# Windowed attention and a gated product on one core: the fifth pass of the first product as short passes in two 64-row halves of the array

## The reference

```python
# x [4, 4096, 192], weight_gen [4, 4096, 8, 7], w_in [192, 2048], w_out [2048, 192]
w = softmax(weight_gen, axis=-1)                      # 7 taps for each of 8 heads
out = np.einsum('bshk,bskhg->bshg', w, x_unf)         # x_unf: the 7 last positions of x, zero padded
x = out.reshape(16384, 192)
h = x @ w_in                                          # first product, contraction over 192
g = h * np.clip(h + 3.0, 0.0, 6.0) / 6.0
return g @ w_out                                      # second product, contraction over 2048
```

## Time and profile before

| | |
|---|---|
| median of 3 runs | 1226.82 us (1226.55 to 1227.56) |
| span of the profiled execution | 1224.4 us |
| median less the span | 2.4 us |
| TensorE busy | 1194.6 us, 98% |
| TensorE weight loads busy | 1083.3 us, 88% |
| VectorE, ScalarE, GpSimd busy | 66%, 52%, 56% |
| granted TensorE clock | 0.999 of full speed |

### The profile page before, as it was taken

How to read it: one execution, slowest core, us unless ns; L and a number is a source line. 1 busy time by engine, 2 the same in 40 slices (tenths; PEclk the granted TensorE clock), 3 DMA queues, 4 the chain that set the end, 5 groups by cost and what they waited for, 6 DMA issues and landing times.

```text
span 1224.4 us, 19650 instructions
## 1 busy us (share of the span) xinstructions
PE 1194.6 (98%) x6848; PEld 1083.3 (88%) x6848; DVE 803.7 (66%) x1362; ACT 634.2 (52%) x1269; POOL 690.8 (56%) x455
## 2 busy tenths in 40 slices
PE   1999999999999999999999999999999999999998
PEld 1899999999999999999999999999999999998997
DVE  7866657576665766656666575766657666566665
ACT  3455555455555555545555554555555555455554
POOL 7893854909358192762918549094581927729100
PEclk9999999999999999999999999999999999999999
DMA  6101010010101001010010100101010010100000
GB/s 179 46 22 58 20 45 13 20 58 20 58 0 65 14 20 58 0 65 13 20 58 20 45 13 20 58 20 58 0 56 22 20 58 0 65 13 13 13 14 13
DMA packets 12071, 42.08 MB, mean 34 GB/s; under 512 B 1183, under 2 KB 5279, under 8 KB 10139
## 3 DMA queue, kind: packets, MB, share of 16 engines
q1 hardware_dynamic: 12059, 41.93, 9.8%
HBM read 29.34 MB, written 12.58 MB: 34 GB/s over the span
## 4 chain that ended last, share of the span: by engine, by line
PE 96%; DVE 1%; POOL 1%; issue 0%; DMA 0%; ACT 0%; DVEq 0%; ACTq 0%
PE work L464 48%; PE sums L482 32%; PE sums L484 15%; PE work L444 2%; POOL pool_acc L154 0%; POOL pool_prod L152 0%; DVE w_in L404 0%; DMA w_raw<-weight_gen_dram 0%; DVE work L350 0%; DVE w_out L410 0%; DVE g_lo L361 0%; DVE out_stage L381 0%; POOL pool_acc L147 0%; POOL pool_prod L148 0%; DVE xt_b L373 0%
## 5 line engine op out<-in xcount | busy, mean ns | idle before, releaser
L350 DVE SCALAR_TENSOR_TENSOR work<-relu,work 128x512 f32<-128x512 f32 x512 | 355.2, 694 | 402.9 <-ACT relu L254 402.8
L482 PE MATMUL sums<-w_out,g_hi 128*128 128x384 f32 x2048 | 614.1, 356 | 0.7 <-DVE g_lo L361 0.7
L254 ACT ACTIVATE relu<-work 128x512 f32<-128x512 f32 x512 | 306.4, 598 | 554.0 <-PE work L464 549.3
L484 PE MATMUL sums<-w_out,g_lo 128*128 128x192 f32 x2048 | 513.0, 251 | 0.0
L464 PE MATMUL work<-xt_a,w_in 128*128 128x512 f32 x1536 | 449.3, 400 | 2.0 <-DVE xt_b L373 2.0
L482 PEld LDWEIGHTS sums<-w_out,g_hi 128*128 128x128 f32 x2048 | 384.3, 188 | 23.7 <-DVE g_lo L361 1.3
L484 PEld LDWEIGHTS sums<-w_out,g_lo 128*128 128x128 f32 x2048 | 389.8, 190 | 15.8
L361 DVE TENSOR_TENSOR g_lo<-work,g_hi 128x512 fp32r<-128x512 f32 x512 | 349.7, 683 | 2.1
L464 PE MATMUL work<-xt_b,w_in 128*128 128x512 f32 x1024 | 318.1, 392 | 0.0
L264 ACT CAST g_hi<-work 128x512 fp32r<-128x512 f32 x512 | 299.3, 585 | 11.4 <-DVE work L350 11.3
L147 POOL TENSOR_TENSOR pool_acc<-x_in,w_soft 128x768 f32<-128x768 f32 (+1 forms) x32 | 50.0, 1563 | 442.7 <-DVE w_soft L341 429.7
(11 more groups left out here) (31 smaller groups left out, 203.7 us busy)
## 6 DMA issues: line engine op xcount, KB each, us to landing
x_in<-x_dram SPq DMA_DIRECT2D x15, 1344.0 KB, 6.0
out_dram<-out_stage SPq DMA_DIRECT2D x32, 384.0 KB, 2.8
w_raw<-weight_gen_dram SPq DMA_DIRECT2D x16, 224.0 KB, 3.0
w_out_raw<-moe_w_out_dram SPq DMA_DIRECT2D x1, 1152.0 KB, 13.5
x_in<-x_dram SPq DMA_DIRECT2D x1, 768.0 KB, 5.1
w_in_raw<-moe_w_in_dram SPq DMA_DIRECT2D x1, 768.0 KB, 8.9
w_in_raw<-moe_w_in_dram SPq DMA_DIRECT2D x2, 384.0 KB, 10.3
w_out_raw<-moe_w_out_dram SPq DMA_DIRECT2D x1, 384.0 KB, 6.6
```

The costliest lines, as they stand in the source:

```text
L254: nc.scalar.activation(t.relu[:, m % 2, :], t.work[m % BANKS][:], ACT.Relu, bias=3.0).then_inc(s.relu_ready, 1)
L350: nc.vector.scalar_tensor_tensor(bank[:], t.relu[:, m % 2, :], 6.0, bank[:], ALU.min, ALU.mult).then_inc(s.gated, 1)
L482: nc.tensor.matmul(t.sums[n][:, 0:2 * D], t.g_hi[:, m % BANKS, cols], t.w_out[:, j, :], start=(j == 0), stop=False)
L484: ins = nc.tensor.matmul(t.sums[n][:, D:2 * D], t.g_lo[:, m % BANKS, cols], t.w_out[:, j, 0:D], start=False, stop=(j == TILES - 1))
```

## The change

The fifth pass (w_lo by the 64 last rows of x) leaves the list of products, which has four passes of 128 rows by 512 columns. In its place, fill of an even slot m issues four short matmuls for the slots m and m + 1 together. Each contracts over 64 rows, the high part of x alone, and covers two of the four token blocks, so 256 columns. Two of them stand behind the first pass of m: blocks 0 and 2 of m from partitions 0 to 63, and blocks 1 and 3 of m + 1 from partitions 64 to 127. The other two stand behind the fourth pass of m: blocks 0 and 2 of m + 1 from partitions 0 to 63, and blocks 1 and 3 of m from partitions 64 to 127. The two of a group use different row halves of the array and different PSUM banks.

Two waits come with it. Since the even slot now writes the bank of m + 1 too, it waits until g_lo of slot m - 3 is written (bank_free). The second group waits on first_smalls, which the last short matmul of the first group counts up. The odd slot has its four passes only, and adds to what its bank holds.

```diff
         products = [(t.w_in[:, 0, 0, cols], t.xt_a[:, half, 0, :]), (t.w_in[:, 0, 0, cols], t.xt_a[:, half, 1, :]),
-                    (t.w_in[:, 1, 0, cols], t.xt_a[:, half, 0, :]), (t.w_in[:, 0, 1, cols], t.xt_b[:, half, :]),
-                    (t.w_in[:, 1, 1, cols], t.xt_b[:, half, :])]
+                    (t.w_in[:, 1, 0, cols], t.xt_a[:, half, 0, :]), (t.w_in[:, 0, 1, cols], t.xt_b[:, half, :])]
+        odd_tile = m % 2 == 1
         for i, (w, x) in enumerate(products):
-            ins = nc.tensor.matmul(bank[:], w, x, start=(i == 0), stop=(i == len(products) - 1))
+            ins = nc.tensor.matmul(bank[:], w, x, start=(i == 0 and not odd_tile), stop=(odd_tile and i == 3))
+            if i == 0 and not odd_tile:
+                if m >= AHEAD:
+                    bank_free(q, m - AHEAD, last)
+                small_product(m, 0, 0, False)
+                small_product(m + 1, 1, 1, False).then_inc(s.first_smalls, 1)
+        if not odd_tile:
+            pe.wait_ge(s.first_smalls, tiles_done(q, m + 1) // 2)
+            small_product(m + 1, 0, 0, False)
+            ins = small_product(m, 1, 1, True)
         ins.then_inc(s.filled, 1)
+
+    def bank_free(q, m, last):
+        if skipped(m, last):
+            return
+        if is_tile(m):
+            pe.wait_ge(s.g_lo_ready, tiles_done(q, m))
+        else:
+            pe.wait_ge(s.xt_lo_ready, inputs_split(q, m))
+
+    def small_product(m, blocks, rows, stop):
+        half, j = slot(m)
+        bank = by_token(t.work[m % BANKS][:], P)[:, blocks::2, :]
+        return nc.tensor.matmul(bank, t.w_in[rows * DB:(rows + 1) * DB, 1, 1, j * P:(j + 1) * P],
+                                block_b(t, half, blocks, rows), start=(m % 2 == 1 and blocks == 1), stop=stop)
```

More of the change, by code:

```diff
@@ L544, in __init__ @@
         self.xt_lo_ready = sem("xt_lo_ready")
+        self.first_smalls = sem("first_smalls")
         self.filled = sem("filled")
```

## The result

The changed kernel takes 1375.87 us (median, 1374.73 to 1376.4), the kernel before 1226.68 us beside it: a ratio of 1.1215, 95% interval 1.1199 to 1.1231. That is 149.2 us more. The forecast was 1408 us, 1168 to 1480.

The account below looks back on a forecast made before the run. TensorE's stream was taken as the bound. A group at 0.823 us, less 0.470 for the two passes before, gives +0.353 us, times 512 +181 us, on 1226.8 us: 1408 us, range 1168 to 1480.

Parts of the forecast that it names:

- Removed passes: Pass 5 of each of the 512 tiles on TensorE goes: 0.235 us each, 120 us, all on the path.
- The choice among cases: Assumed TensorE is emptied at each change between 128 and 64 rows; in all sizes 1269 to 1492 us, chance 0.65.
- pass ahead with its tail: 128-row pass before a group: 0.235 us, plus half its 0.157 us tail, taken as 0.08, before the group starts.
- first load shows: Group's first weight load can't be done ahead behind the running pass, so it shows in full: 0.10 us.
- second load: Weight load of a group's second short pass follows the first load by 0.11 us.
- tail of the short pass: Behind the group, half of the short pass's 0.168 us tail delays the change back to 128 rows: 0.08 us.
- load behind shows: Load of the 128-row matmul behind the group can't be done ahead and shows in full: 0.10 us.
- rival 1: Row changes are free and a group's two short passes run together on TensorE: 1167 to 1180 us; chance 0.26.
- The signs: Profile: change distances above 0.4 us, TensorE idle around groups, loads starting after the pass ahead, 5.2 us per tile pair.
- a case without tails: At row changes only the loads show, no tails: changes of 0.335 us, 0.663 us a group, 1326 us.
- Rival 2: Row changes are free, but a group's second load waits for the first matmul: 1223 to 1232 us; chance 0.07.
- Rival 3: The bank_free wait for g_lo holds the group in every even slot, 197 us: 1424 us; chance 0.02.

Follow-up runs that it names:

- e1: Changed kernel with its short passes contracting over all 128 rows, same places, loads and waits: 1243.12 us, 1.0138 of the kernel before.
- e10: Changed kernel with its short passes contracting over partitions 0 to 95: 1247.39 us, 1.0167 of the kernel before.
- e4: Changed kernel with each group's two short passes issued twice, four in a row: 1433.9 us, 1.1693 of the kernel before.
- e11: Changed kernel with short passes over 32 rows, partitions 0 to 31 and 64 to 95: 1374.56 us, 1.1203 of the kernel before.
- e9: Changed kernel with one short pass per group, that of rows 64 to 127: 1376.48 us, 1.1223 of the kernel before.
- e2: Changed kernel with both short passes of a group in rows 0 to 63: 1433.19 us, 1.1679 of the kernel before.
- e8: Changed kernel with the second group on the first's banks and halves, and no first_smalls wait: 1376.57 us, 1.1229 of the kernel before.
- e12: Changed kernel with four groups behind the first pass of every second pair, on that pair's banks, none elsewhere: 1234.59 us, 1.0068 of the kernel before.
- e5: Changed kernel with both groups side by side behind the even tile's fourth pass, first_smalls wait between them: 1353.34 us, 1.1034 of the kernel before.
- e7: Changed kernel with the first group ahead of the even tile's first pass, behind a 192-column matmul: 1375.65 us, 1.1216 of the kernel before.

## Why the prediction came out as it did

**The bound.** Right: the chain stayed on TensorE, and the whole 149 us came from its stream.

**Removed passes.** 0.235 us each was a little too much: 0.225 by the tiles of four passes.

**The choice among cases.** Right. e1 shows that without the change of rows 133 us go; e10 that it is the change from the whole array to parts of it, not the number of rows; e4 that inside a stretch of short passes nothing of the kind is paid. On both sides of a stretch the matmul in flight holds the next one off for 0.10 us, and the next load, which can't lie beside it, shows for 0.10 us. That the array is emptied is the reading that fits this; the profile has no record of it. The rule of the Trainium skill that the prediction weighed (TensorEngine Tiling (Array Packing), Key Properties: a change of the tiling mode drains the TensorE) agrees with e1 and e11, and with e10 if 96 rows run as the whole array does. Going there and back cost 0.39 to 0.40 us here.

**The terms.** A group was put at 0.823 us from the start of the pass ahead, with what shows behind it. Measured: 0.470 + 149.2 / 512 = 0.761 us. The terms, one by one:

| term | predicted us | measured us | from |
|---|---|---|---|
| pass ahead with its tail | 0.235 + 0.08 | 0.34, 0.33 | timeline |
| first load shows | 0.10 | with the next three in the group's 0.31 to 0.32 | timeline |
| second load | 0.11 | 0 | e9, e2 |
| columns | 0.118 | 0.113 | e4 |
| tail of the short pass | 0.08 | 0.10 (0.315 - 0.113 - 0.10) | e4, if the first load shows for 0.10 |
| load behind shows | 0.10 | 0.09 to 0.10 | timeline |

The mis-sized step is the second load: "the second load follows the first by 0.11 us". It was read from loads of 128 rows that follow each other in the same rows. In two halves the loads lie side by side, two in 0.18 us. Without it the sum would have been 0.713, 1351 us. Both tails were 0.02 us longer than the half that was taken, 0.04 us x 512 = 20 us, and the removed pass saved 0.01 us less, 5 us: 1376 us. The forecast of +181 us was 32 us too high. The two errors ran against each other, and the halves of the tails were a choice between nothing and the whole that no row supported; the measured ones are nearer to two thirds. The stated range, 1168 to 1480 us, also held rival 1, so that 1376 lies in it says little.

**The signs.** A pair of tiles takes 4.57 + 149.2 / 256 = 5.15 us, as forecast (5.2, and above 4.58), and the loads no longer start with the pass ahead. One sign was wrong: the distances at the changes are 0.34, 0.33 and 0.31 us and not above 0.4, and the first two are what the prediction gave for a case without tails (0.335). A load that shows is recorded beside its own matmul, so its 0.10 us lies in the distance behind that start and not ahead of it; the 0.10 us ahead of it are the tail. Nor does TensorE's row show idle time; only that of the loads does.

**Rival 1** had its half right: the two short passes run together (e2, e9), their starts 3 ns apart in the changed kernel's trace. It fell with "no price for the change". **Rival 2** fell on both counts. **Rival 3** fell: with both waits in their places e1 is 133 us faster, and bank_free is hidden in the changed kernel. The other wait, first_smalls, is free too (e8). But "whose place the group takes" was checked at a round's start alone; the tighter place is the slot behind the transposes, where bank_free asks for x_lo instead of g_lo. There it would have cost 10 us had TensorE become as fast as rival 1 wanted, as e12 shows.

## What to carry to other kernels

Using a half of the rows in the middle of a dense stream of full matmuls has a fixed price for each excursion, here 0.39 to 0.40 us or 1.7 passes of 512 columns. It was the same with 192 or 512 columns in flight and with one to eight short passes in the excursion. So collect short work until an excursion holds more than four such pairs (by these prices; no run here gained by it, and with four e12 is at best level), or keep the padded full pass, even if half of its product is waste. In the profile look at idle time of the weight loads put down to "issue" and at distances between starts; TensorE's busy share stays at 98% while it empties. A wait that is free with work between its two ends (e8) costs 0.30 to 0.33 us without (e5).

## What the runs showed of the hardware that was not expected

- Loads for the two halves of the array lie side by side (two in 0.18 us), while two loads for the whole array, or for the same half (two in 0.29 us, e2), start 0.11 us apart.
- 32 rows cost the same as 64 (1374.56 against 1375.87 us), and 96 rows cost nearly what the whole array does (1247.39 us against 1243.12).
- The tail behind 192 columns is that behind 512, 0.09 to 0.11 us (e7).
- A matmul that waits for one just ahead of it in the same queue costs 0.30 to 0.33 us (e5), while the same wait with three long passes between is free (e8).
